# Key and query Grams of a delta-rule attention: zero-padded pairs of heads against one 64-row tile of TensorE per head

## The chip, the cores and the metric

The kernel runs on one core of one Trainium2 chip. TensorE (PE in the profile) multiplies matrices into eight banks of PSUM, VectorE (DVE) and ScalarE (ACT) read PSUM and write SBUF, GpSimd (POOL) works on SBUF, and SyncE (SP) issues all transfers from memory. The metric is the device time of one launch in microseconds (us); less is better.

## What is computed

Three stages follow each other: a linear attention with a delta rule (4 batches, 8 heads, 768 tokens, head dimension 48), a gated block that mixes along the sequence, and a channel mix. Only the first is touched:

```python
k_n = k / (np.linalg.norm(k, axis=-1, keepdims=True) + 1e-06)
for t in range(S):
    y[:, :, t] = np.einsum('bhd,bhde->bhe', q[:, :, t], state)
    v_old = np.einsum('bhde,bhd->bhe', state, kt)
    state = state + bt[:, :, :, None] * np.einsum('bhd,bhe->bhde', kt, vt - v_old)
```

## The kernel before

The attention takes 128 tokens at a time, 24 chunks in all (six per batch). Inside a chunk the recurrence becomes a triangular system: from the Gram matrix of the chunk's keys a 128x128 triangular matrix is made for each head, it is inverted by doubling (levels 1 to 6, blocks of 2, 4, ... tokens), and the inverse times the right side gives the updates, which feed the state and the output.

All loops are written by hand for each engine, and semaphores tie the engines together. One pass of the function `step` does two things interleaved: it **advances** chunk i (solve, state, output) and **prepares** chunk i+1 (Grams, inverse). The first pass only prepares, the last only advances, so 23 passes do both. The eight heads lie in four pairs of 96 = 2 x 48 rows; they are worked in two groups g = 0 and 1 of four heads, each with two PSUM banks: `bank_a[g]` for the key Gram and the inverse, `bank_b[g]` for the keys against the queries and the transposed inverse. Before the change group 0 holds heads 0 to 3 and group 1 heads 4 to 7.

A pass opens with its head stage, which is where the change lies. TensorE's order there is fixed by `step` (L631 and on):

- `gram` (L500 to 509). `part` 0 is keys with keys, `part` 2 is keys with queries. `k_pair` is loaded as weights with both heads of a pair (96 rows), and `moving` holds for each pair four blocks of 128 columns, in which the rows of the other head are zero: `moving[:, p, 0]` has the keys of the pair's first head and zeros below, `moving[:, p, 1]` zeros and the second head's keys, and 2 and 3 the same for the queries. So one matmul of 256 columns gives the Grams of both heads. A group needs two for each part. The zeros are written once, by VectorE for the even buffer and by GpSimd for the odd one, and SyncE waits for them (`zeroed`) before its first loads into each.
- `solve` (L566 to 579), `back` and `correct`: the inverse of a group times the right side, the residual of that, and its correction. The right side is kept in pairs of heads, so each head's matmul streams the 96 columns of its pair and only its own 48 are read, by `own` (L142).
- `start`, `across` and `grow`: the inversion. `queries_with_state`, `add_to_state` and `attend` make output and state and fill TensorE's waits.

VectorE's order in the head stage is `triangles` of group 0 (L327, four instructions, one per head), `read_first` (L362), `triangles` of group 1, `residual` (L367), `updates` (L372), the two `start` multiplications (L335), and then the second group's `read_first` and `residual`. GpSimd makes `ib16` (L243) of each group behind its triangles, and after that `neg_ib`, and masks the scores, which ScalarE has copied out of `bank_b` (L432). SyncE loads the operands of later chunks in `load_grams` (L187 to 194): two loads of keys and two of queries into `moving`, and one into `k_pair`.

Of the kernel before, what the change touches and what calls it, by code (L numbers as in the profile page):

```python
# [19 lines left out]
P = 128  # L20
# [19 lines left out]
def attention(nc, n, dram, keep, bank, weights):  # L40
# [13 lines left out]
    with ctx:  # L54
# [22 lines left out]
        moving = [sb(f"moving{i}", [n.D2, n.NP, 4, P]) for i in range(2)]  # L77
# [25 lines left out]
        zeroed = [sem("zeroed_even"), sem("zeroed_odd")]  # L103
# [19 lines left out]
        gcols = 4 * n.D  # L123

# [16 lines left out]

        def own(b):  # L142

            return b[:, 0:4 * n.D2].rearrange("p (a m c) -> p a m c", m=4, c=n.D)[:, :, 0:4:3, :]

        def own_upd(g):
            return upd[:, 4 * g:4 * g + 4, :].rearrange("p h (e c) -> p (h e) c", e=2).rearrange(
                "p (a m) c -> p a m c", m=4)[:, :, 0:4:3, :]

        def cols(t, g):  # L150
            return t[:, gcols * g:gcols * (g + 1)].rearrange("p (a m c) -> p a m c", m=2, c=n.D)

        def pair_cols(t, h):
            return t[:, (h // 2) * n.D2:(h // 2 + 1) * n.D2]

        def factors(c, i, g):

            return c[:, bass.ds(i, 1), 4 * g:4 * g + 4].rearrange("p o (a m) -> p (o a) m", m=2).unsqueeze(3).to_broadcast(
                [P, 2, 2, n.D])
# [24 lines left out]
        def _(sp):  # L184
            rows_of = dram["k_tok"].rearrange("(i p) m -> p i m", p=P)

            def load_grams(i, par):  # L187

                t = bass.ds(i * P, P)
                for e in range(2):  # L190
                    rows = slice(e * n.D, (e + 1) * n.D)
                    sp.dma_start(moving[par][rows, :, e, :], dram["k_dim"][rows, :, t]).then_inc(grams_in[par], 16)
                    sp.dma_start(moving[par][rows, :, 2 + e, :], dram["q_dim"][rows, :, t]).then_inc(grams_in[par], 16)
                sp.dma_start(k_pair[par][:], dram["k_dim"][:, :, t]).then_inc(grams_in[par], 16)
# [11 lines left out]
            sp.wait_ge(zeroed[0], 1)  # L206
# [4 lines left out]
            sp.wait_ge(zeroed[1], 1)  # L211
# [21 lines left out]
        def _(pool):  # L233
            nc.gpsimd.memset(moving[1][:], 0.0).then_inc(zeroed[1], 1)
# [35 lines left out]
        def _(dve):  # L270
            nc.vector.memset(moving[0][:], 0.0).then_inc(zeroed[0], 1)
# [47 lines left out]
            def triangles(i, g):  # L319
# [5 lines left out]
                for j in range(4):  # L325
                    h = 4 * g + j
                    last = nc.vector.scalar_tensor_tensor(  # L327
                        neg_b[:, h, :], bank_a[g][:, j * P:(j + 1) * P],
# [161 lines left out]
        def _(pe):  # L490
# [76 lines left out]
            def solve(i, par, g):  # L567
# [7 lines left out]
                for h in heads(g):  # L575
                    for part in (rhs_hi, rhs_lo):
                        last = mm(solve_bank[:, (h % 4) * n.D2:(h % 4 + 1) * n.D2], inv_t[par][:, h, :], pair_cols(part, h),
                                  start=h % 4 == 0 and part is rhs_hi, stop=False, skip_group_check=True)
                last.then_inc(first_done, 1)

            def back(i, par, g):
# [3 lines left out]
                for h in heads(g):  # L585
                    last = mm(ks_bank[:, (h % 4) * n.D2:(h % 4 + 1) * n.D2], neg_ib[par][:, h, :], pair_cols(first, h),
                              start=h % 4 == 0, stop=h % 4 == 3, skip_group_check=True)
                last.then_inc(back_done, 1)

            def correct(i, par, g):  # L590

                pe.wait_ge(resid_ready, i * 2 + g + 1)
                for h in heads(g):
# [869 lines left out]
```

## Time and profile before

| | us |
|---|---|
| median of 3 runs | 1082.24 |
| lowest and highest run | 1082.1 and 1086.41 |
| the profiled execution's own span | 1080.0 |

The profile is one execution, taken by the hardware profiler. Its span runs from the first to the last instruction; the runs' times have some 2 us more around it. PE is TensorE's matmuls and PEld its weight loads, which overlap them.
The attention takes the first half of the span: its first Gram starts at 11.4 us, its last transposition at 547.6 us. The stages behind it take the rest, and the diff leaves them alone.

### The profile page before, as it was taken

The page shows a single profiled execution, that of the slowest core. Times are in us where ns is not written, and L with a number is a line of the kernel's source. Part 1 is how long each engine was busy: PE and PEld are TensorE (multiplying, and loading weights), DVE is VectorE, ACT ScalarE, POOL GpSimd, SP SyncE. Part 2 cuts the span into 40 slices and gives each one's busy share as a digit, 9 for nine tenths or more (in the row PEclk, how much of TensorE's full clock was granted, in tenths as well). Part 3 has the DMA queues.
Part 4 walks back from the last instruction along what each step waited for, and adds up shares of the span by engine and source line. Part 5 has one row for each costly group of instructions (what it writes and reads, how often), then busy time and mean ns, then how long its engine had stood idle before and what let it go on. Part 6 is the DMA issues. An engine that isn't in the chain of part 4 may idle for free. (4 is left out here: it accounts for less than half of the span.)

```text
span 1080.0 us, 23381 instructions
## 1 busy us (share of the span) xinstructions
PE 983.5 (91%) x8424; PEld 880.6 (82%) x8424; DVE 615.3 (57%) x1338; ACT 444.4 (41%) x999; POOL 265.5 (25%) x214
## 2 busy tenths in 40 slices
PE   5998879998988989899879999999994899999998
PEld 3787768777877878788768888888884899999998
DVE  5666754667556676666564353443537665555552
ACT  5545543455434554455343231321413434434332
POOL 3344333543335333533621010110204100000000
PEclk8999996999899988999869999999997999999999
DMA  7521231212211111211031000000000000000000
GB/s 220 178 67 44 67 106 31 67 44 67 89 55 58 57 54 53 59 58 53 1 100 69 1 0 0 0 0 0 1 1 1 1 23 22 22 22 22 22 22 22
DMA packets 60388, 47.96 MB, mean 44 GB/s; under 512 B 7104, under 2 KB 58656, under 8 KB 60320
## 3 DMA queue, kind: packets, MB, share of 16 engines
q1 hardware_dynamic: 60320, 47.04, 14.2%
q8 instruction: 44, 0.72, 0.3%
q14 instruction: 24, 0.20, 0.1%
HBM read 42.31 MB, written 4.72 MB: 44 GB/s over the span
## 5 line engine op out<-in xcount | busy, mean ns | idle before, releaser
L441 ACT ACTIVATE inv<-bank 128x256 f16<-128x256 f32 (+1 forms) x288 | 119.2, 420 | 141.5 <-PE bank L538 87.7
L346 DVE TENSOR_TENSOR joined<-bank,level_mask 128x256 f16<-128x256 f32 x288 | 119.3, 423 | 89.3 <-PE bank L523 84.9
L243 POOL TENSOR_TENSOR ib<-neg_b,id 128x512 f16<-128x512 f32 x48 | 60.8, 1267 | 312.6 <-DVE neg_b L327 312.1
L506 PE MATMUL bank<-moving,k_pair 96*128 96x256 f32 x384 | 107.6, 418 | 12.9 <-issue 7.4
L446 ACT ACTIVATE inv_t<-bank 128x256 f16<-128x256 f32 x288 | 94.4, 384 | 9.4 <-PE bank L542 9.4
L506 PEld LDWEIGHTS bank<-moving,k_pair 96*128 96x128 f32 x384 | 74.1, 208 | 23.8 <-issue 8.6
L523 PE MATMUL bank<-inv,ib 128*128 128x64 f16 x1152 | 81.8, 199 | 1.8 <-ACT inv L441 0.6
L542 PE MATMUL bank<-inv_t,joined 128*128 128x64 f16 x1152 | 81.6, 197 | 0.0
L538 PE MATMUL bank<-joined,inv_t 128*128 128x64 f16 x960 | 71.6, 199 | 8.1 <-DVE joined L346 6.5
L711 PE MATMUL bank<-xk_hi,w_k_hi 128*128 128x384 f32 x192 | 65.8, 342 | 12.4 <-DVE xk_lo L1343 12.4
L523 PEld LDWEIGHTS bank<-inv,ib 128*128 128x128 f16 x1152 | 64.3, 104 | 11.9 <-ACT inv L441 3.0
L619 PE MATMUL bank<-upd,scores 128*128 128x96 f32 x384 | 72.2, 303 | 0.4 <-DVE upd L372 0.4
L952 POOL TENSOR_TENSOR rstd<-vareps,neg_half 128x1 f32<-128x1 f32 x24 | 23.7, 987 | 195.3 <-DVE vareps L974 195.3
L1207 ACT ACTIVATE kr<-bank 128x384 f32<-128x384 f32 x64 | 31.2, 489 | 96.0 <-PE bank L713 96.0
L432 ACT ACTIVATE scores<-bank 128x512 f32<-128x512 f32 x48 | 28.5, 596 | 98.9 <-PE bank L506 98.9
L1295 DVE TENSOR_TENSOR sq<-kr 128x384 f32<-128x384 f32 x64 | 38.6, 604 | 53.2 <-ACT kr L1207 53.1
L538 PEld LDWEIGHTS bank<-joined,inv_t 128*128 128x128 f16 x960 | 49.5, 102 | 23.6 <-issue 6.8
L711 PE MATMUL bank<-k_hi,w_v_hi 128*128 128x384 f32 x192 | 64.8, 338 | 3.4 <-DVE k_lo L1300 3.4
L327 DVE SCALAR_TENSOR_TENSOR neg_b<-bank,coef_neg,upper 128x128 f32<-128x128 f32 x192 | 54.2, 344 | 21.5 <-PE bank L506 14.5
L712 PE MATMUL bank<-xk_lo,w_k_hi 128*128 128x384 f32 x192 | 65.3, 340 | 0.0
L713 PE MATMUL bank<-xk_hi,w_k_lo 128*128 128x384 f32 x192 | 65.2, 339 | 0.0
L713 PE MATMUL bank<-k_hi,w_v_lo 128*128 128x384 f32 x192 | 64.7, 337 | 0.0
(144 smaller groups left out, 2460.2 us busy)
## 6 DMA issues: line engine op xcount, KB each, us to landing
k_all<-in_k_tok SPq DMA_DIRECT2D x4, 1152.0 KB, 7.5
moving<-in_k_dim SPq DMA_DIRECT2D x48, 96.0 KB, 2.5
moving<-in_q_dim SPq DMA_DIRECT2D x48, 96.0 KB, 2.5
k_pair<-in_k_dim SPq DMA_DIRECT2D x24, 192.0 KB, 3.0
q_pair<-in_q_dim SPq DMA_DIRECT2D x24, 192.0 KB, 3.0
k_row<-in_k_tok SPq DMA_DIRECT2D x24, 192.0 KB, 2.8
v_row<-in_v_tok SPq DMA_DIRECT2D x24, 192.0 KB, 3.1
out_dram<-o_sb SPq DMA_DIRECT2D x8, 576.0 KB, 2.9
```

Of the source, the lines that this page charges most:

```text
L243: nc.gpsimd.tensor_tensor(group(ib16, g), group(neg_b, g), over_heads(id32[:]), ALU.add).then_inc(b16_ready, 1)
L346: nc.vector.tensor_tensor(blocks(group(joined[:, lv - 1], g), lv, 0), packed(bank_a[g], lv), mask, ALU.mult).then_inc(join_ready, 1)
L441: nc.scalar.activation(to, source, ACT.Copy).then_inc(inv_read, 1)
L446: nc.scalar.activation(blocks(group(inv_t[par], g), lv, 1), packed(bank_b[g], lv), ACT.Copy).then_inc(invt_read[g], 1)
L506: last = mm(to[:, e * 2 * P:(e + 1) * 2 * P], k_pair[par][:, 2 * g + e, :], moving[par][:, 2 * g + e, part:part + 2, :], start=e == 0, sto ...
L523: last = mm(packed(bank_a[g], lv)[:, h % 4], ib16[:, h, :], blocks(inv[:], lv, 0)[:, h], start=h % 4 == 0, stop=h % 4 == 3, skip_group_che ...
L538: last = mm(packed(bank_a[g], lv)[:, h % 4], inv_t[par][:, h, :], blocks(joined[:, lv - 1], lv, 0)[:, h], start=h % 4 == 0, stop=h % 4 == ...
L542: last = mm(packed(bank_b[g], lv)[:, h % 4], joined[:, lv - 1, h, :], blocks(inv_t[par][:], lv, 1)[:, h], start=h % 4 == 0, stop=h % 4 == ...
L619: last = mm(y_bank[:, (h // 2) * n.D2:(h // 2 + 1) * n.D2], scores[par][:, h, :], upd[:, h, :], start=False, stop=h == n.H - 1, skip_group ...
L711: mm(out, sh, mh, start=first and i == 0, stop=False)
L712: mm(out, sh, ml, start=False, stop=False)
L713: ins = mm(out, sl, mh, start=False, stop=last and i == len(pairs) - 1)
```

## The change

The zero blocks go. `kq` takes the place of `moving`: 128 partitions, in which the first head of each pair lies in rows 0 to 47 and the second in rows 64 to 111, keys in block 0 and queries in block 1. Each head then has matmuls of its own, of 48 rows and 128 columns, with its own keys as weights; the program gives them TensorE tiles of 64 rows by 128 columns, at row 0 or row 64. For that each of the two row tiles gets banks of its own, so the groups are now the first heads of the pairs (0, 2, 4, 6) and the second heads (1, 3, 5, 7). `gram` does all eight heads of a part at once. In `solve`, `back` and `correct` each head streams its own 48 columns instead of its pair's 96. VectorE's reads of these results become contiguous, and its writes to `first`, `resid` and `upd` strided. `k_pair` is still loaded, for the state. The memsets of the zeros and SyncE's two waits for them are gone. `attend` now waits for the scores of both groups.

```diff
-        moving = [sb(f"moving{i}", [n.D2, n.NP, 4, P]) for i in range(2)]
+        kq = [sb(f"kq{i}", [P, n.NP, 2, P]) for i in range(2)]
...
+        def tile_of(h):
+            return 4 * (h % 2) + h // 2
+
         def own(b):
-
-            return b[:, 0:4 * n.D2].rearrange("p (a m c) -> p a m c", m=4, c=n.D)[:, :, 0:4:3, :]
+            return b[:, 0:4 * n.D].rearrange("p (a c) -> p a c", c=n.D)
...
-                    rows = slice(e * n.D, (e + 1) * n.D)
-                    sp.dma_start(moving[par][rows, :, e, :], dram["k_dim"][rows, :, t]).then_inc(grams_in[par], 16)
-                    sp.dma_start(moving[par][rows, :, 2 + e, :], dram["q_dim"][rows, :, t]).then_inc(grams_in[par], 16)
+                    rows, to = slice(e * n.D, (e + 1) * n.D), slice(e * P // 2, e * P // 2 + n.D)
+                    sp.dma_start(kq[par][to, :, 0, :], dram["k_dim"][rows, :, t]).then_inc(grams_in[par], 16)
+                    sp.dma_start(kq[par][to, :, 1, :], dram["q_dim"][rows, :, t]).then_inc(grams_in[par], 16)
...
-            sp.wait_ge(zeroed[0], 1)
             load_grams(0, 0)
...
-            nc.gpsimd.memset(moving[1][:], 0.0).then_inc(zeroed[1], 1)
...
-            nc.vector.memset(moving[0][:], 0.0).then_inc(zeroed[0], 1)
...
-            def gram(i, par, i2, g, part):
-
-                if part == 0 and g == 0:
+            def gram(par, i2, part):
+
+                if part == 0:
                     pe.wait_ge(grams_in[par], i2 * 80 + 80)
-                to = (bank_b if part else bank_a)[g]
-                for e in range(2):
-                    last = mm(to[:, e * 2 * P:(e + 1) * 2 * P], k_pair[par][:, 2 * g + e, :],
-                              moving[par][:, 2 * g + e, part:part + 2, :], start=e == 0, stop=e == 1,
-                              skip_group_check=True)
-                last.then_inc(kq_done if part else gram_done, 1)
+                for p in range(n.NP):
+                    for e in range(2):
+                        rows = slice(e * P // 2, e * P // 2 + n.D)
+                        last = mm((bank_b if part else bank_a)[e][:, p * P:(p + 1) * P], kq[par][rows, p, 0, :],
+                                  kq[par][rows, p, part, :], start=p == 0, stop=p == n.NP - 1, skip_group_check=True)
+                        if p == n.NP - 1:
+                            last.then_inc(kq_done if part else gram_done, 1)
...
-                    last = mm(ks_bank[:, (h % 4) * n.D2:(h % 4 + 1) * n.D2], neg_ib[par][:, h, :], pair_cols(first, h),
-                              start=h % 4 == 0, stop=h % 4 == 3, skip_group_check=True)
+                for j in range(4):
+                    last = mm(ks_bank[:, j * n.D:(j + 1) * n.D], neg_ib[par][:, 4 * g + j, :], head_cols(first, g, j),
+                              start=j == 0, stop=j == 3, skip_group_check=True)
...
-                pe.wait_ge(scores_ready, i * 2 + some[-1] // 4 + 1)
+                pe.wait_ge(scores_ready, i * 2 + 2)
...
                 if prepare:
-                    gram(q, nxt, i2 + par, 0, 0)
+                    gram(nxt, i2 + par, 0)
                 if advance:
                     solve(i, par, 0)
                 if prepare:
-                    gram(q, nxt, i2 + par, 1, 0)
 
                     if advance:
                         pe.wait_ge(invt_read[1], (i + 1) * (NL - 1))
-                    gram(q, nxt, i2 + par, 0, 2)
+                    gram(nxt, i2 + par, 1)
                 if advance:
                     back(i, par, 0)
-                if prepare:
-                    gram(q, nxt, i2 + par, 1, 2)
-                if advance:
                     correct(i, par, 0)
```

TensorE, in the head stage of a pass that does both, from the end of `solve` of group 0 on, before the change (`_lo` and `_hi` are the two halves of the right side):

```order
L577 MATMUL bank<-rhs_lo,inv_t 128x96
L506 MATMUL bank<-moving,k_pair 128x256 x2
L506 MATMUL bank<-moving,k_pair 128x256 [waits invt_read_second]
L506 MATMUL bank<-moving,k_pair 128x256
L583 ISA
L584 REGISTER_ALU [waits ib_ready]
L586 MATMUL bank<-first,neg_ib 128x96 [waits first_read]
L586 MATMUL bank<-first,neg_ib 128x96 x3
L506 MATMUL bank<-moving,k_pair 128x256 x2
L594 MATMUL bank<-resid,inv_t 128x96 [waits resid_ready]
```

Two Gram matmuls of 256 columns stand ahead of `solve` (not shown), four behind it, and two between `back` (L586) and `correct` (L594).

The same place after the change:

```order
L571 MATMUL bank<-rhs_lo,inv_t 128x48
L500 MATMUL bank<-kq 128x128 [waits invt_read_second]
L500 MATMUL bank<-kq 128x128 x7
L577 ISA
L578 REGISTER_ALU [waits ib_ready]
L580 MATMUL bank<-first,neg_ib 128x48 [waits first_read]
L580 MATMUL bank<-first,neg_ib 128x48 x3
L588 MATMUL bank<-resid,inv_t 128x48 [waits resid_ready]
```

The key Grams of the second group have moved ahead of `solve`, where eight matmuls of 128 columns stand now; behind it all eight keys-with-queries matmuls stand together, and nothing is left between `back` and `correct`.

## Rows read from the trace of the kernel before

**Rows 1.** The page: span; busy time, share, instructions; clock in 40 slices, in tenths.
```profile
span 1080.0 us, 23381 instructions
PE 983.5 (91%) x8424; PEld 880.6 (82%) x8424; DVE 615.3 (57%) x1338; ACT 444.4 (41%) x999; POOL 265.5 (25%) x214
...
PEclk8999996999899988999869999999997999999999
```

**Rows 2.** Busy time per stretch: hot head stage, cold head stage, hot pass; clock.
```profile
core 0: us, PE busy (x) PEld busy (x) DVE busy (x) ACT busy (x) POOL busy (x), PEclk, DMA share, GB/s
321.34:330.96 9.62, 8.15 (x70) 6.96 (x69) 6.76 (x17) 3.19 (x7) 6.88 (x6) 1.00 0.22 63
161.42:176.60 15.18, 15.00 (x68) 12.92 (x69) 5.54 (x14) 2.39 (x4) 8.58 (x7) 0.50 0.08 22
321.00:341.20 20.20, 18.43 (x248) 16.10 (x246) 13.24 (x33) 10.48 (x29) 8.60 (x7) 1.00 0.20 60
```

**Rows 3.** Timeline of TensorE in the hot head stage: start, us, instruction, [idle before].
```profile
321.34 1.03 PE L506 MATMUL bank<-moving,k_pair 96*128 96x256 f32 x4
322.55 0.20 PE L577 MATMUL bank<-rhs_hi,inv_t 128*128 128x96 bf16 x1 [0.19 <-DVE rhs_lo L357]
...
322.89 1.96 PE L506 MATMUL bank<-moving,k_pair 96*128 96x256 f32 x8
324.69 1.03 PE L586 MATMUL bank<-first,neg_ib 128*128 128x96 f32 x8
325.55 1.06 PE L506 MATMUL bank<-moving,k_pair 96*128 96x256 f32 x4
326.44 0.34 PE L594 MATMUL bank<-resid,inv_t 128*128 128x96 bf16 x4
...
329.58 0.40 PE L515 MATMUL bank<-id,inv_t 128*128 128x128 f16 x4 [1.01 <-DVE inv_t L335]
...
330.96 0.40 PE L523 MATMUL bank<-inv,ib 128*128 128x64 f16 x8
```

**Rows 4.** Timeline of VectorE in the same stretch.
```profile
321.85 0.56 DVE L357 TENSOR_TENSOR rhs_lo<-rhs,rhs_hi 128x384 bf16<-128x384 f32 x1
322.51 1.13 DVE L327 SCALAR_TENSOR_TENSOR neg_b<-bank,coef_neg,upper 128x128 f32<-128x128 f32 x4
323.56 0.35 DVE L362 COPY first<-bank 128x192 f32<-128x192 f32 x1
324.14 1.13 DVE L327 SCALAR_TENSOR_TENSOR neg_b<-bank,coef_neg,upper 128x128 f32<-128x128 f32 x4 [0.23 <-PE bank L506]
325.75 0.35 DVE L367 TENSOR_TENSOR resid<-rhs,bank 128x192 bf16<-128x192 f32 x1 [0.49 <-PE bank L586]
326.91 0.36 DVE L372 TENSOR_TENSOR upd<-bank,coef 128x192 f32<-128x192 f32 x1 [0.80 <-PE bank L594]
327.18 2.35 DVE L335 TENSOR_TENSOR inv_t<-ib,first_mask 128x512 f16<-128x512 f16 x2
```

**Rows 5.** Timeline of GpSimd in the same stretch.
```profile
323.72 1.26 POOL L243 TENSOR_TENSOR ib<-neg_b,id 128x512 f16<-128x512 f32 x1 [11.22 <-DVE neg_b L327]
```

**Rows 6.** Groups by shape, 55 to 490 us: count, busy us and mean ns, idle before.
```profile
L523 PE MATMUL bank<-inv,ib 128*128 128x64 f16 x960 | 67.4, 197 | 0.9
L586 PE MATMUL bank<-first,neg_ib 128*128 128x96 f32 x320 | 46.0, 291 | 0.0
```

**Rows 7.** Timeline of TensorE in the cold head stage.
```profile
161.42 2.07 PE L506 MATMUL bank<-moving,k_pair 96*128 96x256 f32 x4 [3.71 <-issue]
163.93 3.75 PE L506 MATMUL bank<-moving,k_pair 96*128 96x256 f32 x8
...
169.13 1.97 PE L506 MATMUL bank<-moving,k_pair 96*128 96x256 f32 x4
```

**Rows 8.** Timeline of the opening, all engines.
```profile
1.23 1.76 DVE L271 MEMSET moving<- 96x2048 f32 x1 [1.23 <-PEq L1456]
...
14.94 2.16 DVE L327 SCALAR_TENSOR_TENSOR neg_b<-bank,coef_neg,upper 128x128 f32<-128x128 f32 x8
```

More of the change, by code:

```diff
@@ L140, in over_heads, with head_cols @@
             return m.unsqueeze(1).to_broadcast([P, 4, P])
+        def tile_of(h):
+            return 4 * (h % 2) + h // 2
         def own(b):
[L144 removed]
+            return b[:, 0:4 * n.D].rearrange("p (a c) -> p a c", c=n.D)
         def own_upd(g):
[L147 to L148 removed]
+            return upd[:, g:n.H:2, g * n.D:(g + 1) * n.D]
         def cols(t, g):
[L151 to L154 removed]
+            return t.rearrange("p (a e c) -> p a e c", e=2, c=n.D)[:, :, g, :]
+        def head_cols(t, g, j):
+            return t[:, (2 * j + g) * n.D:(2 * j + g + 1) * n.D]
         def factors(c, i, g):
[L158 to L159 removed]
+            return c[:, bass.ds(i, 1), g:n.H:2].rearrange("p o a -> p (o a)").unsqueeze(2).to_broadcast([P, 4, n.D])
         def every_chunk(eng, step):
@@ L574, in solve @@
                     pe.wait_ge(upd_ready, i * 2 + 1)
-                for h in heads(g):
+                for j in range(4):
                     for part in (rhs_hi, rhs_lo):
-                        last = mm(solve_bank[:, (h % 4) * n.D2:(h % 4 + 1) * n.D2], inv_t[par][:, h, :], pair_cols(part, h),
-                                  start=h % 4 == 0 and part is rhs_hi, stop=False, skip_group_check=True)
+                        last = mm(solve_bank[:, j * n.D:(j + 1) * n.D], inv_t[par][:, 4 * g + j, :], head_cols(part, g, j),
+                                  start=j == 0 and part is rhs_hi, stop=False, skip_group_check=True)
                 last.then_inc(first_done, 1)
@@ L584, in back @@
                 pe.wait_ge(first_read, i * 2 + g + 1)
-                for h in heads(g):
-                    last = mm(ks_bank[:, (h % 4) * n.D2:(h % 4 + 1) * n.D2], neg_ib[par][:, h, :], pair_cols(first, h),
-                              start=h % 4 == 0, stop=h % 4 == 3, skip_group_check=True)
+                for j in range(4):
+                    last = mm(ks_bank[:, j * n.D:(j + 1) * n.D], neg_ib[par][:, 4 * g + j, :], head_cols(first, g, j),
+                              start=j == 0, stop=j == 3, skip_group_check=True)
                 last.then_inc(back_done, 1)
@@ L592, in correct @@
                 pe.wait_ge(resid_ready, i * 2 + g + 1)
-                for h in heads(g):
-                    last = mm(solve_bank[:, (h % 4) * n.D2:(h % 4 + 1) * n.D2], inv_t[par][:, h, :], pair_cols(resid, h),
-                              start=False, stop=h % 4 == 3, skip_group_check=True)
+                for j in range(4):
+                    last = mm(solve_bank[:, j * n.D:(j + 1) * n.D], inv_t[par][:, 4 * g + j, :], head_cols(resid, g, j),
+                              start=False, stop=j == 3, skip_group_check=True)
                 last.then_inc(solved, 1)
@@ L615, in attend @@
                 pe.wait_ge(upd_ready, i * 2 + 2)
-                pe.wait_ge(scores_ready, i * 2 + some[-1] // 4 + 1)
+                pe.wait_ge(scores_ready, i * 2 + 2)
                 for h in some:
-                    last = mm(y_bank[:, (h // 2) * n.D2:(h // 2 + 1) * n.D2], scores[par][:, h, :], upd[:, h, :],
+                    last = mm(y_bank[:, (h // 2) * n.D2:(h // 2 + 1) * n.D2], scores[par][:, tile_of(h), :], upd[:, h, :],
                               start=False, stop=h == n.H - 1, skip_group_check=True)
```

7 lines of the change are left out of this document (2 added, 5 removed).

## The prediction

> **What bounds the kernel now.** I read the page first: the span is 1080.0 us, TensorE is busy 91% of it [rows 1]. That share is an average and says nothing of the head stage, where the change lies, so I went to the busy time by stretch. A pass at the upper clock level takes 20.20 us, and its head stage, from the first Gram to the first `across`, 9.62 us of it [rows 2]. There are 23 such passes; the stretch at 321 us stands for them. In the head stage TensorE is busy 8.15 of 9.62 us, VectorE 6.76: neither fills it, so I laid the timelines of both side by side, counting from the first Gram at 321.34 = 0.
>
> TensorE: key Grams of group 0 at 0; `solve` at 1.21, held until `rhs_lo` is written; eight instructions of Gram at 1.55; `back` at 3.35; the last Grams at 4.21; `correct` at 5.10; later it idles 1.01 us for `start` and issues that at 8.24; the first `across` stands at 9.62 [rows 3]. VectorE: `rhs_lo` ends at 1.07; triangles of group 0 at 1.17 to 2.30; `first` at 2.22; triangles of group 1 at 2.80 after 0.23 us of idling for their Gram; `resid` at 4.41 after 0.49 us for `back`; `upd` at 5.57 after 0.80 us for `correct`; the two `start` multiplications at 5.84 to 8.19 [rows 4]. So one chain alternates between the engines. VectorE sets it where it works (triangles, `start`), and TensorE's Grams sit in the gaps: `back` comes late because of the Grams ahead of it, `correct` because of those between it and `back`. From `start` at 5.84 to the end of the head stage nothing depends on a Gram any more. The gain or loss per pass is therefore how far the time 5.84 moves.
>
> **The change, term by term.**
>
> *Gram instructions.* Before, a pass has 16 of 256 columns. Two rows of four and eight of them take 1.03 and 1.96 us, so four more cost 0.93, 0.23 each [rows 3]. After, there are 32 of 128 columns, 16 per part. Upper bound for one: `back`, with the same weights' width of 128 and fewer columns (96), has (1.03 - 0.29) / 7 = 0.106 us between starts [rows 3, 6], and half of 0.23 is 0.115. A row of 96 columns needs only 0.09 by that rate, so the 128-column weight load sets the 0.106. In one row after another, 16 thus take 1.7 to 1.8 us, and all 32 take 3.4 to 3.7, what the 16 wide ones take now. Lower bound: the two heads of a pair lie in different rows of the array and write different banks; if both streams and both weight loads run side by side, it is half, 0.053, and 16 take 0.85, or 0.96 with the first and last alone (9 slots of 0.106). Issuing is no lower limit: 64-column matmuls start every (0.40 - 0.20) / 7 = 0.03 us [rows 3, 6]. No row of this trace has two matmuls of different row tiles. I take the lower bound, since disjoint rows and banks leave nothing visible that they must share; the other end is the first rival. The Trainium skill, "TensorE: Matmul & The Clock Gate", Part 3, says that matmuls in different row groups run concurrently and that weight loads overlap when the row groups differ; no row here shows it.
>
> *Changing the array's shape.* The Grams' 64-row shape stands between 128-row shapes on both sides, four changes a pass. If each change waits until the array is empty, it costs about the tail of the last matmul, its duration less the distance of starts: 0.29 - 0.106 = 0.18 for `back`, 0.20 - 0.03 = 0.17 for the short ones [rows 3, 6]. Bounds: 0 and 0.2. I take 0.2, the costly end, because all matmuls before had one row shape and the overlap they show is no evidence for mixed ones. The Trainium skill, "TensorEngine Tiling (Array Packing)", Key Properties, speaks against the change here: "Changing tiling mode (not just tile) drains the TensorE"; by that rule the costly end holds, without it each pass gains 0.2 us more.
>
> *The head stage laid out anew* (both values taken). Key Grams of all heads 0.2 to 1.16, results at 1.35, so the triangles start at 1.35 instead of 1.17 and end at 2.48. `solve` 1.36 to 1.6 (the right side was ready at 1.07); keys with queries 1.8 to 2.76; `first` 2.48 to 2.83; triangles of group 1 2.83 to 3.96. `back` 2.96 (instead of 3.35) to 3.81, result at 4.0. It streams 48 columns instead of 96 but keeps its pace, since the weight load sets 0.106. `resid` 4.1 to 4.45, `correct` 4.55 to 4.85, `upd` 4.95 to 5.25, `start` at 5.25. Against 5.84 that is **0.6 us less per pass**. The cover between `back` and `correct` is gone: TensorE now idles there from 3.81 to 4.55, and this is what stops the gain; with free switches I get 5.05, 0.8 us less. GpSimd has `ib16` of group 0 done at 2.5 + 1.3 = 3.8 and of group 1 at 4.05 + 1.3 = 5.35 [rows 5], ahead of the two `start` instructions at 5.25 and 6.45, so it does not take over. From there VectorE's 2.35 us and what follows move as one block.
>
> *Short solves.* 24 matmuls of 96 bf16 columns become 48; each saves some 0.01 (from 0.04 to the 0.03 above), but only `correct`'s four stand on the path, 0.05 us, already in the sum.
>
> *Cold passes.* In one head stage the granted clock is 0.50 throughout, and it takes 15.18 us with TensorE busy 15.00 [rows 2]: there TensorE alone is the bound. Its Grams take 2.07 + 3.75 + 1.97 = 7.8 us, less three tails of some 0.3 [rows 7], so 7 us; half of that, 3.5, goes, and four switches of 0.25 and a bare wait behind `back` come: 2.5 us less. The page's clock line shows two more low places in the attention (the 8s in slices 11 and 15 to 16) [rows 1]; I count two heads as half cold, at 1.2 us each. The idle 3.71 us ahead of the Gram [rows 7] is not the change's; it waits for nothing shown, where a loop turns back. A pass gets 16 more matmuls and 16 more loads; I cost the longer stream at nothing, as issue keeps up at 0.03 us. If such gaps grew by a tenth, it would be some 1 us in all.
>
> *The opening.* The memset of 1.76 us and the wait for it leave the front. The triangles of the first chunk start only at 14.94, where the coefficients made from `k_all` are ready, and do not hang on the Grams [rows 8]. Gain up to the memset's 1.76 us where the constants come earlier, loss of as much if the earlier Gram loads hold up `k_all`; I take 0.
>
> *At nothing:* the DMAs have the same sizes and count; strided VectorE writes replace strided reads; `attend` waits for scores that were masked a pass ago; ScalarE's copies of scores get theirs at 3 us, it is idle then.
>
> **Sum:** 20 passes x 0.6 = 12.0, the full cold one 2.5, two half cold ones 2.4, together 16.9. 1080.0 - 16.9 = 1063.1 us of span, and with the 2.2 us by which the median stands above it: **1065 us**. Its own range: free switches give 20 x 0.8 + 5.5 = 21.5, or 1061, with a faster opening and luck with gaps 1055; half of the gain gives 1074.
>
> **Rivals.**
>
> *Tiles that load in single file.* If weight loads of the two tiles take turns (0.106 each), nothing is saved. For it: the loads, not the columns, set `back`'s pace, and there are twice as many loads now. Without switches: Grams to 1.7, results 1.95, triangles at 2.0 to 3.13, `first` to 3.48, `back` at 3.75, `start` near 5.95, a loss of 0.1 that earlier `correct`s give back: **1082**, no change.
>
> *Single file and switches, slower.* The same with 0.2 a switch: results at 2.2, triangles to 3.33, keys with queries 2.7 to 4.4, `back` 4.65 to 5.5, `resid` 5.75, `start` 6.85: 1.0 us more in each of 23 passes, **1105**. It turns from gain to loss where a Gram instruction takes about 0.085 us.
>
> *The clock.* The head stage becomes emptier: TensorE's work there falls from 8.15 to some 6 us. The trace has the clock at 0.50 in stretches that follow idle gaps (the 3.71 us ahead of the cold Gram), and keeps 1.00 through a 1.01 us wait for `start` [rows 2, 3, 7]. If the longer idling drops it, a cold head stage costs 15.18 - 2.5 = 12.7 against 9.62, 3.1 us more. Set against the gains, it takes 5 of the 20 hot passes to eat them all; with all 20, 1080 + 62 - 5 + 2 = **1139**. Against it: hot passes hold their clock with that wait in each.
>
> **How the numbers follow.** Forecast (side by side, switches or not) 0.50; between the bounds, near 1074, 0.10; single file without switches 0.15; single file with switches 0.13; clock 0.12. A measurement of this kernel tells about 0.5% (5.4 us) from no change. Faster: 0.50 + 0.09 = 0.59; slower: 0.13 and most of the clock's, 0.24; within: 0.17. The range runs from 1054 to 1103: it leaves out the slow end of the second rival and most of the clock's case.
>
> **What would show it.** Right: in the hot head stage 16 Gram instructions span 1.0 to 1.3 us with starts in near pairs; `back` starts near 3.0 and `start` near 5.2; a hot pass takes 19.6; `resid` is still awaited, and TensorE idles before `correct`. A span of 1.8 us for a part shows single file; a gap of 0.2 before each change of shape shows the switch; a clock of 0.50 in passes that follow no gap shows the third rival. Wrong would also be a VectorE instruction (`first`, `resid`, `upd`) above 0.40 us: three of them lie on the path twice over.

## The result: slower, by 0.9%

| | us |
|---|---|
| kernel before, median of 5 runs | 1082.10 |
| changed kernel, median of 5 runs | 1090.76 |
| ratio, 95% interval | 1.0093 (1.0062 to 1.0124) |
| span of the changed kernel's profiled execution | 1089.0 |

The forecast was 1065 us. The Grams do what the change says; the time is lost elsewhere. The page of the changed kernel, against [rows 1] (span; busy time, share and instructions; granted clock in 40 slices):

```profile
span 1089.0 us, 24147 instructions
PE 993.8 (91%) x8808; PEld 903.8 (83%) x8808; DVE 599.3 (55%) x1337; ACT 441.6 (41%) x999; POOL 265.0 (24%) x213
...
PEclk9987786887868878888869999999997999999999
```

TensorE is busier than before, though it got less to do, and the clock line shows why: where before most slices of the attention stand at 9, now most stand at 7 or 8. In the trace's record of the granted clock 23 stretches at 0.50 begin between 40 us and 545 us, 212 us in all; in the kernel before there are 9, 78 us in all. Behind 570 us the two lines are nearly alike.

TensorE in a head stage of the changed kernel, from the timeline (start, us, instruction, idle before), against [rows 3]:

```profile
121.13 1.16 PE L500 MATMUL bank<-kq 48*128 48x128 f32 x16
122.54 1.16 PE L500 MATMUL bank<-kq 48*128 48x128 f32 x16
124.02 1.09 PE L580 MATMUL bank<-first,neg_ib 128*128 128x48 f32 x8 [0.31 <-DVE first L355]
125.56 0.27 PE L588 MATMUL bank<-resid,inv_t 128*128 128x48 bf16 x4 [0.45 <-DVE resid L360]
...
128.13 0.40 PE L509 MATMUL bank<-id,inv_t 128*128 128x128 f16 x4 [1.01 <-DVE inv_t L328]
...
128.65 1.83 PE L580 MATMUL bank<-first,neg_ib 128*128 128x48 f32 x8
130.28 0.63 PE L517 MATMUL bank<-inv,ib 128*128 128x64 f16 x8
```

Sixteen Gram instructions take 1.16 us. With one at 0.27 that is 0.06 from start to start, half of the 0.115 that the prediction gave for one after another. Counting from the first Gram, `back` starts at 2.89, `correct` at 4.43, the second `start` at 7.00 instead of 8.24. Up to there the pass is 1.2 us ahead of the one before. Then the second `back` takes 1.83 us, where the first took 1.09, and the eight `across` take 0.63 instead of 0.40: the clock has fallen. VectorE and GpSimd in the same stretch, against [rows 4, 5]:

```profile
122.43 1.27 DVE L320 SCALAR_TENSOR_TENSOR neg_b<-bank,coef_neg,upper 128x128 f32<-128x128 f32 x4 [0.32 <-PE bank L500]
123.62 0.34 DVE L355 COPY first<-bank 128x192 f32<-128x192 f32 x1
123.88 1.11 DVE L320 SCALAR_TENSOR_TENSOR neg_b<-bank,coef_neg,upper 128x128 f32<-128x128 f32 x4
125.15 0.35 DVE L360 TENSOR_TENSOR resid<-rhs,bank 128x192 bf16<-128x192 f32 x1
125.98 0.36 DVE L365 TENSOR_TENSOR upd<-bank,coef 128x192 f32<-128x192 f32 x1 [0.47 <-PE bank L588]
126.25 1.83 DVE L328 TENSOR_TENSOR inv_t<-ib,first_mask 128x512 f16<-128x512 f16 x2
...
126.30 2.90 POOL L239 TENSOR_TENSOR neg_ib<-neg_b,id 128x512 f32<-128x512 f32 x2
```

The pair of `start` multiplications (L328) begins at 5.12 instead of 5.84, and takes 1.83 us instead of 2.35. The forecast had the first of these (5.25) and not the second. In the kernel before GpSimd's first `neg_ib` had begun 0.61 us ahead of the pair; here it begins 0.05 behind it (before, the first instruction of each):

```profile
327.18 0.94 DVE L335 TENSOR_TENSOR inv_t<-ib,first_mask 128x512 f16<-128x512 f16 x1
```

```profile
326.57 1.27 POOL L245 TENSOR_TENSOR neg_ib<-neg_b,id 128x512 f32<-128x512 f32 x1
```

The busy time by stretch for a whole pass, and for the part of it in which the clock stands at 0.50 (columns as in [rows 2]):

```profile
99.73:120.67 20.94, 19.27 (x252) 17.71 (x249) 11.66 (x31) 9.37 (x26) 8.67 (x7) 0.76 0.19 57
...
105.00:112.00 7.00, 6.18 (x59) 5.63 (x58) 3.16 (x8) 2.51 (x6) 5.38 (x5) 0.50 0.00 0
```

In the pass shown further above, the clock falls behind the second `start`, for which TensorE had waited 1.01 us; in this one it has fallen by 105 us, about the time of the first `start`. It stays at 0.50 for some 7 us in most passes, and a pass takes 20.9 to 21.2 us. Before, it was 20.2 [rows 2].

The opening is slower too: the first transposition stands at 56.8 us instead of 52.6. The triangles start at 15.12 instead of 14.94 [rows 8]; the rest is most likely clock. The trace's record of the clock begins only at 50.1 us here, so the digits of the page's first two slices say nothing, but the matmuls show it: at 30 us a row of four 64-column ones takes 0.40 us, 0.28 in a hot stretch, and at 33.6 us sixteen Gram instructions take 2.08, 1.16 in a hot stretch. The record of the kernel before has 0.50 from 20.6 to 27.4 us and from 41.1 to 44.5, and 1.00 from 17.2 to 20.6 and between the two:

```profile
15.12 2.16 DVE L320 SCALAR_TENSOR_TENSOR neg_b<-bank,coef_neg,upper 128x128 f32<-128x128 f32 x8
...
30.04 0.40 PE L536 MATMUL bank<-inv_t,joined 128*128 128x64 f16 x4
...
33.59 2.08 PE L500 MATMUL bank<-kq 48*128 48x128 f32 x16
```

So 4.2 us come from the opening, in which the first pass that does both is counted, 6.3 from the 23 passes between the first and the last transposition (22 that do both, and the one that only advances), and 1.5 are won behind them: 9.0 us of span. The 6.3 is itself a difference. 14 of these passes took 20.0 to 20.4 us before; they are 13.3 us longer now, 0.95 each. The other nine, of which eight had a stretch at 0.50 before too, are 7.0 us shorter in all.

### The profile page after: what moved, and what is told of

It is laid out like the page before. It is cut to its first block and busy times, and to the rows that moved or that the text cites. A ratio compares the mean times of both kernels' runs of the same rounds, so it can differ in the third digit from the quotient of the medians.

```text
span 1089.0 us, 24147 instructions
## 1 busy us (share of the span) xinstructions
PE 993.8 (91%) x8808; PEld 903.8 (83%) x8808; DVE 599.3 (55%) x1337; ACT 441.6 (41%) x999; POOL 265.0 (24%) x213
## 5 line engine op out<-in xcount | busy, mean ns | idle before, releaser
L517 PE MATMUL bank<-inv,ib 128*128 128x64 f16 x1152 | 92.0, 214 | 2.3 <-ACT inv L434 0.6
L536 PE MATMUL bank<-inv_t,joined 128*128 128x64 f16 x1152 | 88.5, 207 | 0.0
L517 PEld LDWEIGHTS bank<-inv,ib 128*128 128x128 f16 x1152 | 75.6, 117 | 12.1 <-ACT inv L434 5.3
L532 PE MATMUL bank<-joined,inv_t 128*128 128x64 f16 x960 | 78.3, 211 | 4.5 <-DVE joined L339 3.4
L580 PEld LDWEIGHTS bank<-first,neg_ib 128*128 128x128 f32 x384 | 70.1, 273 | 10.2 <-issue 6.5
L580 PE MATMUL bank<-first,neg_ib 128*128 128x48 f32 x384 | 73.3, 352 | 5.8 <-DVE first L355 5.8
L500 PE MATMUL bank<-kq 48*128 48x128 f32 x768 | 63.6, 310 | 15.2 <-DMA k_pair<-in_k_dim 8.1
L532 PEld LDWEIGHTS bank<-joined,inv_t 128*128 128x128 f16 x960 | 57.8, 111 | 17.5 <-issue 4.4
L500 PEld LDWEIGHTS bank<-kq 48*128 48x128 f32 x768 | 53.4, 209 | 21.9 <-issue 11.5
L239 POOL TENSOR_TENSOR neg_ib<-neg_b,id 128x512 f32<-128x512 f32 x48 | 69.2, 1461 | 0.0
```

The source lines that it names most:

```text
L500: last = mm((bank_b if part else bank_a)[e][:, p * P:(p + 1) * P], kq[par][rows, p, 0, :], kq[par][rows, p, part, :], start=p == 0, stop=p ...
L517: last = mm(packed(bank_a[g], lv)[:, h % 4], ib16[:, h, :], blocks(inv[:], lv, 0)[:, h], start=h % 4 == 0, stop=h % 4 == 3, skip_group_che ...
L532: last = mm(packed(bank_a[g], lv)[:, h % 4], inv_t[par][:, h, :], blocks(joined[:, lv - 1], lv, 0)[:, h], start=h % 4 == 0, stop=h % 4 == ...
L536: last = mm(packed(bank_b[g], lv)[:, h % 4], joined[:, lv - 1, h, :], blocks(inv_t[par][:], lv, 1)[:, h], start=h % 4 == 0, stop=h % 4 == ...
L580: last = mm(ks_bank[:, j * n.D:(j + 1) * n.D], neg_ib[par][:, 4 * g + j, :], head_cols(first, g, j), start=j == 0, stop=j == 3, skip_group ...
```

## The experiments

Two questions stood at the start. Does the clock fall because TensorE has less to do in the head stage (A), or because of the instructions' new shape (B)? And where does the rest of what the head stage gained come from (1.24 us up to the second `start`, 0.6 forecast)? All runs in one table: the ratio is to runs of the kernel before on the same chip; "pass" is the shortest time from transposition to transposition without a low clock (the last pass of the attention left out), or the median of all where nearly every pass has one (*); "low" is the number of stretches at 0.50 that begin between 40 and 545 us, and their sum; "start" the mean time of one `start` multiplication.

| run | median us | ratio (95%) | pass us | low | start us |
|---|---|---|---|---|---|
| before | 1082.1 | 1 | 20.2 | 9, 78 us | 1.20 |
| changed | 1090.8 | 1.009 (1.006 to 1.012) | 21.1* | 23, 212 | 0.97 |
| e1_filler | 1053.7 | 0.974 (0.967 to 0.981) | 18.8 | 5, 75 | 0.99 |
| e2_tiles_wide | 1099.6 | 1.018 (1.011 to 1.025) | 21.7* | 22, 126 | 1.47 |
| e3_narrow | 1100.6 | 1.020 (1.015 to 1.026) | 21.1* | 22, 126 | 1.26 |
| e4_bf16 | 1086.1 | 1.006 (1.002 to 1.010) | 19.7 | 12, 109 | 1.46 |
| e5_before_fill | 1075.2 | 0.993 (0.989 to 0.996) | 20.2 | 6, 65 | 1.20 |
| e6_narrow_fill | 1084.6 | 1.004 (0.999 to 1.009) | 20.0 | 5, 72 | 1.26 |
| e7_fill_late | 1065.3 | 0.987 (0.978 to 0.996) | 18.9 | 19, 109 | 0.96 |
| e8_fill_early | 1064.2 | 0.981 (0.975 to 0.987) | 18.9 | 18, 116 | 0.98 |
| e9_one_tile | 1111.7 | 1.026 (1.017 to 1.035) | 20.7 | 14, 123 | 1.18 |
| e10_full_shape | 1089.4 | 1.006 (1.002 to 1.010) | 20.5 | 4, 41 | 1.33 |
| e11_more_fill | 1053.7 | 0.972 (0.964 to 0.979) | 18.9 | 5, 61 | 0.97 |
| e12_fill_pool_waits | 1035.4 | 0.960 (0.952 to 0.967) | 18.0 | 7, 61 | 0.42 |
| e13_wide_pool_waits | 1030.6 | 0.952 (0.946 to 0.959) | 18.0 | 6, 61 | 0.42 |
| e14_before_pool_waits | 1033.4 | 0.955 (0.948 to 0.963) | 18.6 | 5, 41 | 0.42 |
| e15_after_pool_waits | 1047.1 | 0.970 (0.965 to 0.974) | 17.8 | 15, 130 | 0.42 |

### Work in the idle places

```diff
+            def fill(width):
+                mm(state_bank[0:n.D2, 0:width], zeros[:, 0:n.D2], zeros[:, 0:width], start=False, stop=False,
+                   skip_group_check=True)
...
                     back(i, par, 0)
+                    if prepare:
+                        fill(192)
                     correct(i, par, 0)
...
                     start(q, nxt, 0)
+                    if advance:
+                        fill(384)
                     start(q, nxt, 1)
```

> The changed kernel with two extra float32 matmuls per pass that add zeros to the state bank: 192 columns between `back` and `correct` of group 0, 384 columns between the two `start`s of the inversion, both in places where TensorE idles. Theory A (the clock falls because TensorE has too little to do in the head stage): the regular stretches at 0.50 go or become rare, mean clock 0.93 or more, a hot pass 19.4 us, in all 1060 to 1070 us. Theory B (it falls because the new instructions are narrow, 48 rows or 48 columns, whatever the idle time): clock stays at 0.89 to 0.90, time 1090 or more.

1053.7 us, and a pass at full clock takes 18.9. The busy time of such a pass, and the two fills (L627) in TensorE's timeline:

```profile
352.70:371.60 18.90, 17.86 (x268) 15.26 (x266) 12.62 (x33) 10.37 (x29) 8.69 (x7) 1.00 0.21 62
```

```profile
356.87 0.53 PE L627 MATMUL bank<-zeros 128*96 128x192 f32 x2
...
358.86 0.84 PE L627 MATMUL bank<-zeros 128*96 128x384 f32 x2
360.03 0.40 PE L509 MATMUL bank<-id,inv_t 128*128 128x128 f16 x4 [0.34 <-DVE inv_t L328]
```

Both stand where TensorE idled and delay nothing: the second `start` comes at 6.90 us after the first Gram, with 0.34 us of waiting left. All narrow instructions are still there, so B as stated (the clock stays low whatever else TensorE does) falls. The regular low stretches are gone, five are left, most of them behind the loops' gaps. The time is below the range forecast for A (1060 to 1070 us), since a hot pass takes 18.9 us and not 19.4.

Each fill alone, and two more fills (96 columns ahead of `back`, 96 behind the late one):

> The changed kernel with only the later fill (384 columns, between the two `start`s). If any added work in the head stage will do: regular stretches at 0.50 gone as with both fills, 1048 to 1060 us. If both are needed: some passes fall, 1062 to 1085 us.

> The changed kernel with only the earlier fill (192 columns between `back` and `correct`). The later fill alone took the low stretches from 23 of 7 us and more to 19 shorter ones and gave 0.9865. If the amount of added work counts, half as much work as the later one leaves nearly every pass with a stretch at 0.50: 1075 to 1088 us. If the place counts (between the Grams and `start`, ahead of where the clock falls), it does as well as the later one or better: 1055 to 1067 us.

> The changed kernel with the two fills and two more of 96 columns, one ahead of `back` of group 0 and one behind the 384 columns. If the clock needs yet more work in the head stage to leave its stretches at 0.50 behind the loops' gaps sooner: fewer of these stretches than 5, 1040 to 1050 us. If those stretches have nothing to do with the fills: 1050 to 1058 us, as with two; where the first of the new fills delays `back`, up to 1062 us.

Either fill alone leaves 18 or 19 low stretches, but most are 3.4 us long instead of 7, and both give about 1065 us. The early one, half as wide, does as much as the late one. Two more fills beyond the two change nothing (1053.7): more work in the head stage doesn't remove the low stretches that stay.

### The parts of the change, one at a time

Only the narrow solves, in the kernel before:

```diff
         def pair_cols(t, h):
-            return t[:, (h // 2) * n.D2:(h // 2 + 1) * n.D2]
+            return t[:, h * n.D:(h + 1) * n.D]
...
-                    last = mm(ks_bank[:, (h % 4) * n.D2:(h % 4 + 1) * n.D2], neg_ib[par][:, h, :], pair_cols(first, h),
+                    last = mm(ks_bank[:, (h % 4) * n.D:(h % 4 + 1) * n.D], neg_ib[par][:, h, :], pair_cols(first, h),
```

> The kernel before with only the narrow solves: `solve`, `back` and `correct` stream each head's own 48 columns, Grams and groups as before. Theory A: head stage hardly emptier (some 0.3 us of 8.15), clock as before at 0.94 to 0.95, 1077 to 1083 us. Theory B, if it is the 48 columns: clock falls in nearly every pass to 0.90, 1090 to 1100 us.

> The narrow solves alone (the run e3_narrow) with the later fill of 384 columns. If e3_narrow was slow by an emptier head stage: the regular stretches at 0.50 go, mean clock 0.94 or more, 1070 to 1080 us. If narrow instructions themselves lower the clock: it stays at 0.90 to 0.91 and 1098 us or more.

Theory A's number for e3 was wrong, and what B had said for it came out: 1100.6 us, 22 low stretches, a mean clock of 0.91 over the run. This edit touches no Gram, and `back` still starts every 0.1 us:

```profile
244.32 0.99 PE L586 MATMUL bank<-first,neg_ib 128*128 128x48 f32 x8
```

```profile
240.73:261.70 20.97, 18.99 (x246) 17.01 (x245) 13.25 (x33) 10.52 (x28) 8.60 (x7) 0.92 0.19 56
```

Yet it alone tips nearly every pass (mean clock 0.92 in this one). With the late fill (e6) the low stretches are 5 and the pass 20.0 us, so it isn't the narrow instruction alone either. The kernel before holds its clock by little: each of the three thinnings of the head stage that were tried (e2, e3 and, in part of the passes, e4) loses it. What e6 gains per pass, 0.1 to 0.2 us, doesn't show in its time, 1.004 (0.999 to 1.009); at 1084.6 us it missed both of its ranges.

Only the row tiles: each head of the changed kernel streams its pair's 96 columns again.

```diff
-        def own(b):
-            return b[:, 0:4 * n.D].rearrange("p (a c) -> p a c", c=n.D)
+        def own(b, g):
+            return b[:, 0:4 * n.D2].rearrange("p (a e c) -> p a e c", e=2, c=n.D)[:, :, g, :]
...
         def head_cols(t, g, j):
-            return t[:, (2 * j + g) * n.D:(2 * j + g + 1) * n.D]
+            return t[:, j * n.D2:(j + 1) * n.D2]
```

> The changed kernel with `solve`, `back` and `correct` back at 96 columns (each head streams its pair's columns), row tiles for the Grams kept. Theory A: TensorE's work in the head grows by only about 0.2 us, the clock still falls once in nearly every pass, 1086 to 1093 us. Theory B, if it is the 48 columns: the clock holds, 1063 to 1070 us. Theory B, if it is the 48-row tiles: as A.

1099.6 us, outside all the ranges given, and slower than the changed kernel although it has the shorter low stretches. VectorE and GpSimd show a second thing:

```profile
243.89 2.85 DVE L330 TENSOR_TENSOR inv_t<-ib,first_mask 128x512 f16<-128x512 f16 x2
```

```profile
243.78 2.67 POOL L239 TENSOR_TENSOR neg_ib<-neg_b,id 128x512 f32<-128x512 f32 x2
```

The two `start` multiplications take 2.85 us here, 1.83 in the changed kernel. There VectorE came 0.05 us ahead of GpSimd's `neg_ib`, here 0.11 behind.

Thinner Grams without row tiles, in bf16 and the old order:

```diff
-                    last = mm(to[:, e * 2 * P:(e + 1) * 2 * P], k_pair[par][:, 2 * g + e, :],
-                              moving[par][:, 2 * g + e, part:part + 2, :], start=e == 0, stop=e == 1,
-                              skip_group_check=True)
+                    for _ in range(2):
+                        last = mm(to[:, e * 2 * P:(e + 1) * 2 * P], k_pair[par][:].bitcast(bf16)[:, 2 * g + e, 1::2],
+                                  moving[par][:].bitcast(bf16)[:, 2 * g + e, part:part + 2, 1::2], start=e == 0,
+                                  stop=e == 1, skip_group_check=True)
```

> The kernel before with its Grams in bf16 (the upper halves of the float32 words), each issued twice, so that 16 instructions of 256 columns take some 0.11 us each instead of 0.23; 96 rows, no row tiles, 96-column solves, old order. The second pair's Grams of each group come out doubled. TensorE's Gram work is halved as in the changed kernel, by another way. Theory A: the clock falls in most passes, 0.88 to 0.91, 1080 to 1092 us. Theory B: the clock holds at 0.94 or more and the time is 1062 to 1070 us.

In between: 12 low stretches, 1086.1 us. Less Gram work lowers the clock in part of the passes without any row tile. The start pair is slow here too (2.9 us), and takes back part of what the Grams give.

The late fill in the kernel before:

> The kernel before with only the later of the two fills: a float32 matmul of 384 columns that adds zeros to the state bank, between the two `start`s, where TensorE idles 1.0 us. If the fill helped the changed kernel only by undoing what the change did to the clock, it gives nothing here: 1075 to 1082 us, a hot pass stays 20.2 us. If the fill is a gain of its own (fewer or shorter stretches at 0.50 behind the loops' gaps), 1060 to 1072 us, and part of the 2.6% belongs to it.

0.993 (0.989 to 0.996): nearer to "nothing". What the late fill is worth in the changed kernel is the clock that the change had lost, but for this 0.7%. The early fill was not tried in the kernel before.

### Are the tiles what makes the Grams fast, and what does the change of shape cost?

Both runs of this part have the two fills. In the first, all heads lie in rows 0 to 47:

```diff
-        kq = [sb(f"kq{i}", [P, n.NP, 2, P]) for i in range(2)]
+        kq = [sb(f"kq{i}", [n.D, n.NP, 4, P]) for i in range(2)]
...
-                        last = mm((bank_b if part else bank_a)[e][:, p * P:(p + 1) * P], kq[par][rows, p, 0, :],
-                                  kq[par][rows, p, part, :], start=p == 0, stop=p == n.NP - 1, skip_group_check=True)
+                        last = mm((bank_b if part else bank_a)[e][:, p * P:(p + 1) * P], kq[par][:, p, 2 * e, :],
+                                  kq[par][:, p, 2 * e + part, :], start=p == 0, stop=p == n.NP - 1, skip_group_check=True)
```

> The changed kernel with both fills, but both heads of a pair lie in rows 0 to 47, so all Gram matmuls use the same row tile of 64. If it was the two row tiles that made the Grams fast: 16 instructions take 1.7 to 1.9 us instead of 1.16, `back` starts 0.5 us later or more, a hot pass 19.4 to 19.9 us instead of 18.9, 1064 to 1080 us. If 48-row matmuls are quick by themselves: 1.16 us and 1050 to 1058 us.

The next run has `kq` with 96 rows and zeros again, and `k_pair` as weights, one matmul per head:

> The changed kernel with both fills, each head with its own matmuls of 128 columns, but in the 128-row shape: the pair's 96 rows as weights, the other head's rows of the moving side zero, as in the kernel before. No row tiles and no change of shape. Against the one-tile run it differs by the shape changes alone. If those are what costs: 16 Gram instructions in 1.8 us with no gap behind them, a hot pass 19.6 to 20.0 us, 1065 to 1080 us. If a run of matmuls in one file costs the same either way: a hot pass 20.7 us as with one tile, 1090 us or more.

TensorE with one row tile, then in the full shape (the Grams of part 0, the first `solve`, the Grams of part 2):

```profile
60.45 2.05 PE L499 MATMUL bank<-kq 48*128 48x128 f32 x16
62.43 0.20 PE L570 MATMUL bank<-rhs_hi,inv_t 128*128 128x48 bf16 x1
...
62.73 2.05 PE L499 MATMUL bank<-kq 48*128 48x128 f32 x16
```

```profile
79.52 2.05 PE L503 MATMUL bank<-kq,k_pair 96*128 96x128 f32 x16
81.41 0.19 PE L574 MATMUL bank<-rhs_hi,inv_t 128*128 128x48 bf16 x1
...
81.61 2.03 PE L503 MATMUL bank<-kq,k_pair 96*128 96x128 f32 x16
```

Without a second tile, 16 take 2.05 us, 0.12 apart, whatever the shape (1.7 to 1.9 us had been expected). So the two tiles run side by side, weight loads included, and that is the 0.06. `solve` stands 1.98 us behind the first Gram with one tile and 1.89 in the full shape, the next Grams 0.30 and 0.20 behind `solve`: a change of shape costs 0.1 us, and `back` comes 4.26 and 3.96 us after the first Gram. Without the tiles, the new order takes 20.5 us per pass even at full clock, against 20.2 before; part of this is the `start` pair: one multiplication takes 1.33 us there and 1.20 before.

The two runs also say something of the clock. e9 was forecast at 1064 to 1080 us and took 1111.7, e10 1089.4, though their Grams take the same time and their full-clock passes are only 0.2 us apart. e9 has 14 low stretches, e10 has 4. And in e9 the clock falls where TensorE had not been idle at all, at 107.2 us for instance, in the middle of the head stage:

```profile
101.50:107.20 5.70, 5.70 (x57) 5.25 (x56) 3.83 (x12) 2.21 (x5) 2.00 (x2) 1.00 0.37 104
```

That stretch holds the 32 Gram instructions of 48 rows from one tile. In e10, with 96 rows, the same place at the same pace keeps 1.00. So idle time can't be all that counts, and theory B stays alive in a weaker form: an instruction that uses fewer rows (or, after e3, fewer columns) seems to hold the clock less, however long it keeps TensorE busy. The fills can't tell the two apart, since they add both busy time and columns.

### The two engines that stood in each other's way

```diff
+                pool.wait_ge(start_ready, i * 2 + 2)
                 for g in range(2):
                     nc.gpsimd.tensor_tensor(group(neg_ib[par], g), group(neg_b, g), over_heads(id32[:]),
                                             ALU.subtract).then_inc(ib_ready, 1)
```

This one wait lets VectorE's pair go first. It was put into four kernels: the one before (e14), e2 (e13), the changed kernel with an early and a late fill of 192 columns each (e12), and the changed kernel alone (e15).

> The kernel before with the wait on GpSimd alone. Theory L: the pair takes 0.83 instead of 2.35 us, 1.4 us less per pass, hot pass 18.8 us, 1046 to 1058 us; then more than half of what the changed kernel's hot passes gained beyond the forecast is this, and it can be had without row tiles. Otherwise 1078 to 1084 us.

> Row tiles with 96-column solves (the run e2_tiles_wide) and the same wait on GpSimd. There the pair takes 2.85 us, and VectorE came 0.1 us behind `neg_ib`; in the changed kernel it came 0.05 us ahead of it and the pair takes 1.83. Theory L: 0.83 us here too, 2.0 us less per pass; 1048 to 1062 us with the clock of e2_tiles_wide. Otherwise 1094 to 1104 us as there, and the 96 columns themselves would be what made that run slower than the changed kernel.

> The changed kernel with an early fill of 192 columns and a late one of 192 (not 384), and GpSimd waits for both `start` multiplications of VectorE before it makes `neg_ib`. In the changed kernel the pair of multiplications takes 1.83 us, the first 0.41 and the second 1.4, beside `neg_ib`. Theory L (the two engines take turns at SBUF, the one that comes first goes first): the pair takes 0.83 us, a hot pass 17.9 to 18.3 us instead of 18.9, 1028 to 1042 us. If the multiplication is slow for another reason (its input comes late): the pair stays at 1.8, 1052 to 1058 us.

> The changed kernel with the wait on GpSimd and nothing else, no fills. The kernel before with this wait has a hot pass of 18.6 us and row tiles with 96-column solves and this wait 18.0 us, both with six or fewer stretches at 0.50. If the shorter wait between the two `start`s fills the head stage enough: hot pass 17.9 to 18.0 us, the clock holds (0.95 or more), 1026 to 1036 us. If the 48-column solves again tip it: one stretch at 0.50 in most passes, mean clock 0.90 to 0.93, 1040 to 1060 us.

VectorE and GpSimd in the kernel before with the wait, then a pass by stretch, of it and of the tiles with 96-column solves:

```profile
96.05 0.75 DVE L336 TENSOR_TENSOR inv_t<-ib,first_mask 128x512 f16<-128x512 f16 x2
```

```profile
96.88 2.51 POOL L246 TENSOR_TENSOR neg_ib<-neg_b,id 128x512 f32<-128x512 f32 x2 [1.40 <-DVE inv_t L336]
```

```profile
71.20:89.84 18.64, 18.32 (x247) 16.11 (x246) 11.63 (x33) 10.35 (x28) 8.29 (x7) 1.00 0.21 63
```

```profile
74.20:92.20 18.00, 17.13 (x264) 15.21 (x260) 11.58 (x33) 10.21 (x29) 8.29 (x7) 1.00 0.22 66
```

A multiplication takes 0.42 us in all four and the pair 0.75 us, against 2.35, 2.85 or 1.83. A plain wait on GpSimd makes the kernel before 4.5% faster; `neg_ib` has time until the next pass. The hot pass gets shorter by what the pair does, 1.6 us. The effect on the time was larger than forecast (1033 instead of 1046 to 1058); there are also fewer low stretches, 5 instead of 9. With it out of the way, the row tiles are worth 18.64 - 18.00 = 0.64 us a pass, the forecast's 0.6, but the times of the two runs, 0.955 and 0.952, can't be told apart: from the first to the last transposition e13 takes 6.4 us less than e14 (440.9 against 447.4), and its opening takes 3.6 us more. And the changed kernel as it stands plus the wait, e15, is 1047.1: it has the shortest passes of all (17.8 us), and 15 low stretches that make about half of them 20.0. Between it and e13 lies only the width of the solves. GpSimd's rate differs as well: `neg_ib` takes 2.5 us alone and 2.7 to 2.9 beside VectorE.

Single instructions show how. In the kernel before, the first `neg_ib` ends at 326.57 + 1.27 = 327.84 us, and VectorE's first multiplication, which had begun at 327.18, at 328.12, 0.28 behind. In e2 it also ends 0.28 us behind the GpSimd instruction that had begun ahead of it, and takes 1.44 us. In the changed kernel it comes first and takes 0.42; GpSimd's takes 1.49 instead of 1.27, and the second multiplication, now behind, ends 0.28 us after that. So the one that starts later seems to wait for the whole of the other.

The Trainium skill, "SBUF — State Buffer", Who interferes with whom, says that a VectorE instruction with two SBUF inputs contends with a GpSimd instruction that reads SBUF, and that "Issue order, not op shape, decides who blocks." The traces agree: 0.05 us ahead or 0.11 behind makes 1.83 or 2.85 us of the same pair.

## Why the prediction was wrong, step by step

- **Grams.** Right. It took the lower bound, 16 in 0.96 and the tail of the last one; measured 1.16 with the tail, or 0.06 apart. The first rival, single file, is excluded, and e9 shows what it would have cost.
- **Change of shape.** The mechanism is right, its size was put too high: 0.2 each, measured 0.1, and none that shows ahead of the first Grams, where e9 and e10 begin alike.
- **The head stage laid out anew.** `back` forecast at 2.96, measured 2.89; `correct` 4.55 and 4.43; `start` 5.25 and 5.12. VectorE's strided writes cost nothing (0.34 to 0.36 us).
- **"From there VectorE's 2.35 us and what follows move as one block."** Wrong. The pair of `start`s is not a fixed block: it took 1.83 in the changed kernel because it came just ahead of GpSimd. This gave another 0.5 us per pass, by luck of 0.05 us: with the 0.7 by which 5.84 moved, a hot pass got 1.3 us shorter (18.9, read from e1) where 0.6 was forecast. The text took GpSimd only as a producer of `ib16` ("so it does not take over"), not as one that competes.
- **The clock.** This is the step that failed: the sum has every hot pass stay hot (20 x 0.6), and the rival that says otherwise got 0.12. "Against it: hot passes hold their clock with that wait in each" took a wait that was survived as a sign of reserve. The rival's place was right and its price too high: it had a whole head stage at 0.50, 3.1 us a pass; here a stretch of 7 us that begins late in the head stage costs 21.1 - 18.9 = 2.2 us, in nearly every pass. Against the 1.3 us that were won (20.2 - 18.9) this makes 0.9 a pass. The rival also named idling as the cause; e1 fits that, e3 hardly (TensorE is busy 7.78 of 9.46 us in a hot head stage, against 8.15 of 9.62 before) and e9 doesn't. And the forecast held the narrow solves for nothing but 0.05 us; e3 shows that they alone tip the clock, 2.0% of the time.
- **Cold passes and loops' gaps.** The pass with the wholly cold head took 30.6 us from transposition to transposition (157.2 to 187.8 us), and takes 27.7 now, 2.9 less where 2.5 was forecast. Its counterpart half-way through went the other way, from 25.1 to 29.0 us. Four half cold ones, not two, got shorter by 1.5 each (22.8 and 24.7 us before, 21.2 and 23.25 now). And of the 23 passes before, 15 were hot throughout, not 20.
- **The opening.** Forecast 0, measured 4.2 us slower, most likely by the clock that rises later. Why it rises later was not tested. The 17 traces have a pattern: the clock's first stretch at 1.00 begins at 15.6 to 17.2 us in the six kernels whose float32 Grams use 96 rows (before, e3, e5, e6, e10, e14), and at 29.7 us or later in the eleven whose Grams use 48 rows or are bf16.
- **Range.** 1054 to 1103 held 1090.8, the likeliest case and its sign did not.

## What to carry to other kernels

Before work is taken off TensorE, look at whether its clock holds by a margin: a kernel in which a stage with waits runs at 1.00 may fall when its next 32 matmuls get narrower, and what follows in the pass pays for it. Test this with matmuls that add zero in the idle places before the change is judged, and don't take a busy engine for a safe one: e9 lost its clock without idling. And where VectorE and GpSimd both work on SBUF, look at the same instruction's duration in several kernels; if it differs, decide by a wait which of the two goes first.

## What the runs showed that was not expected

- One wait on GpSimd is worth 4.5% (e14), five times the size of the change's own effect. The trace of before hinted at it by the duration: 1.20 us for a multiplication that takes 0.42 alone.
- Matmuls of 192 and 384 columns that add zeros, 0.53 and 0.84 us of a pass, make the changed kernel 37 us faster (1090.8 to 1053.7).
- The clock can fall while TensorE is busy without a break, if its matmuls use 48 rows (e9), and holds at the same pace with 96 (e10).
- Two row tiles of 64 take float32 matmuls with 128-column weights at 0.06 us each, against 0.12 from one tile. Changing between the 64-row and the 128-row shape costs 0.1 us.
- What remains open: by what the clock is decided between e13 (6 low stretches) and e15 (15), which differ in the streamed width of 32 matmuls a pass (24 in bf16, 8 in float32), how much rows, columns and idle time each count (e9 and e10 differ in the 64-row and the 128-row shape too, and ran on different chips), and why one early fill does as much as a late one of twice its width.
